# A recurrence, two mixture stages and a greedy routing on one core: the first two turns laid out anew, and the row numbers of an expert found a step sooner

## The reference, cut to what matters

```
for t in range(768):                       # 4 batches x 8 heads, head size 48
    y[t]  = r[t] . (state + u*k[t] (x) v[t])
    state = w[t]*state + k[t] (x) v[t]
x  = y as 3072 tokens x 384
h  = x @ w_in                              # 384 -> 2048
g  = h * tanh(softplus(h))
x2 = g @ w_out                             # 2048 -> 384
logits = x2 @ w_gate                       # 8 experts
# greedy routing: (token, expert) pairs by falling logit; a token keeps its
# first expert, an expert takes 384 tokens at most
out[tokens of e] = relu(x2[tokens of e] @ w1[e]) @ w2[e]
```

## Time and profile before

| | us |
|---|---|
| median of 3 runs (798.05 to 803.17) | 799.06 |
| the profiled execution | 798.34 |
| its span, first to last instruction | 796.6 |
| PE busy | 769.7 (97%) |
| DVE busy | 628.6 (79%) |
| ACT, POOL busy | 425.1, 292.7 |

### The profile page before, as it was taken

One profiled execution on the slowest core, in us unless ns is written; L12 is line 12 of the kernel. 1 busy time (PEld: TensorE's weight loads), 2 busy tenths in 40 slices (PEclk: granted clock), 3 DMA queues, 4 the chain that ended last, 5 costly groups with the idle time before them and its releaser, 6 DMA issues.

```text
span 796.6 us, 17145 instructions
## 1 busy us (share of the span) xinstructions
PE 769.7 (97%) x6810; PEld 577.1 (72%) x6810; DVE 628.6 (79%) x1081; ACT 425.1 (53%) x703; POOL 292.7 (37%) x244
## 2 busy tenths in 40 slices
PE   8899999999999999999999999987999999999994
PEld 8888878787878787878787877655565665666662
DVE  8969999999998999998999985877776767766220
ACT  2478759595968595868686779410121221222221
POOL 4424482627272727272726350011221231222311
PEclk9999999999999999999999999995999999999998
DMA  9962266464656464655464347114423415415500
GB/s 306 377 210 64 78 201 245 144 237 142 233 187 213 151 230 159 212 210 196 170 208 174 117 154 248 61 53 157 172 90 148 188 61 189 187 44 207 218 31 30
DMA packets 47791, 133.49 MB, mean 168 GB/s; under 512 B 5344, under 2 KB 19808, under 8 KB 45664
## 3 DMA queue, kind: packets, MB, share of 16 engines
q1 hardware_dynamic: 38880, 93.07, 33.7%
q0 software_dynamic: 5376, 34.61, 11.8%
q10 hardware_dynamic: 3456, 4.72, 1.7%
HBM read 97.78 MB, written 34.60 MB: 166 GB/s over the span
## 4 chain that ended last, share of the span: by engine, by line
PE 83%; DVE 10%; issue 2%; DMA 2%; ACT 2%; POOL 0%; SPq 0%; DVEq 0%
PE bank L425 80%; DVE cmp L1316 2%; DMA stage<-in_moe_w_out 1%; DVE g_lo L1416 1%; ACT t_sb L807 1%; PE bank L730 1%; PE bank L450 1%; PE bank L511 1%; DVE inv L1008 1%; DMA k_tok<-in_k 1%; DVE t_sb L1395 1%; DVE rdec L1023 0%; DVE t_sb L1388 0%; DVE t_sb L1391 0%; DVE thr L1333 0%
## 5 line engine op out<-in xcount | busy, mean ns | idle before, releaser
L425 PE MATMUL bank<-x_hi,win_hi 128*128 128x256 f16 (+1 forms) x588 | 158.8, 272 | 1.6 <-DVE h_sb L1080 0.9
L425 PE MATMUL bank<-x_lo,win_hi 128*128 128x256 f16 (+1 forms) x588 | 158.7, 272 | 0.0
L425 PE MATMUL bank<-x_hi,win_lo 128*128 128x256 f16 (+1 forms) x588 | 158.7, 272 | 0.0
L1547 POOL TENSOR_TENSOR g_lo<-t_sb,g_hi 128x512 f16<-128x512 f32 x88 | 122.3, 1420 | 47.0 <-ACT g_hi L807 47.0
L425 PE MATMUL bank<-wout_hi,g_hi 128*128 128x392 f16 (+1 forms) x416 | 129.0, 317 | 0.0
L425 PE MATMUL bank<-wout_lo,g_hi 128*128 128x392 f16 (+1 forms) x416 | 128.8, 316 | 0.0
L425 PE MATMUL bank<-wout_hi,g_lo 128*128 128x392 f16 (+1 forms) x416 | 128.7, 316 | 0.0
L807 ACT ACTIVATE g_lo<-bank 128x384 f16<-128x384 f32 x64 | 31.4, 490 | 144.1 <-PE bank L425 124.7
L1530 POOL TENSOR_TENSOR dv<-v_tok,dot 128x384 f32<-128x384 f32 x24 | 29.8, 1240 | 186.7 <-DVE dot L1038 186.7
L807 ACT ACTIVATE g_hi<-t_sb 128x512 f16<-128x512 f32 x96 | 56.5, 624 | 54.6 <-PE bank L425 54.4
L1087 DVE TENSOR_TENSOR t_sb<-t_sb,h_sb 128x512 f32<-128x512 f32 x96 | 83.0, 913 | 2.0 <-ACT t_sb L807 1.4
(11 more groups left out here) (184 smaller groups left out, 1593.7 us busy)
## 6 DMA issues: line engine op xcount, KB each, us to landing
stage<-in_moe_w SPq DMA_DIRECT2D x22, 768.0 KB, 6.5
w_split<-stage SPq DMA_DIRECT2D x22, 768.0 KB, 4.5
fold_w<-in_moe_w SPq DMA_DIRECT2D x10, 768.0 KB, 8.9
w_split<-fold_w SPq DMA_DIRECT2D x10, 768.0 KB, 7.6
wt<-in_w_turned SPq DMA_DIRECT2D x24, 258.0 KB, 2.8
kt<-in_k_turned SPq DMA_DIRECT2D x24, 256.0 KB, 2.6
rt<-in_r_turned SPq DMA_DIRECT2D x24, 256.0 KB, 2.8
r_tok<-in_r SPq DMA_DIRECT2D x24, 192.0 KB, 6.0
```

What stands on the lines that cost most here:

```text
L425: return nc.tensor.matmul(*a, **k)
L1547: G.tensor_tensor(g_lo[:, j * GW:(j + 1) * GW], t_sb[:, j * GW:(j + 1) * GW], g_hi[:, j * GW:(j + 1) * GW], ALU.subtract).then_inc(s["glo" ...
```

## The change

- **PE, turns 0 and 1.** The blocks of folded products go: `fold_one` puts single ones between the matmuls of tiles (0,4), (0,5), (0,7), (1,3), (1,4) and of three half tiles, 42 in all, and 6 stand at the end of turn 0. `values(2)` goes between the matmuls of tile (0,6). The first halves of turn 1's tiles 0, 1 and 2 are made at the end of turn 0, as they need only chunk 2's x; `values(3)` goes between the matmuls of two of them. `scores(2)` moves behind tile (0,4). In turn 1 chunk 5's steps come two slots later.
- **DVE, turns 0 and 1.** A new list. `gated(0, 1)` to `gated(0, 7)` move from the end of turn 0 into slots 0 to 5 of turn 1, `split_piece(2)` moves ahead of `inverse(2, 0)`, `split_piece(4)` and `(5)` into turn 0. `copied` of turn 1 waits also for the product of the same part of h.
- **ACT, turns 0 and 1.** `rounded(0, ...)` moves into turn 1's slots 0 to 6, ahead of the copies; in turn 0 the pieces 4 and 5 come two slots later, and chunk 3's keys and x among the sines. POOL's `remainder(0, ...)` follow, and its piece 3 waits for one more DVE piece.
- **Second stage.** `PLACES`, DVE's loop and the idle products:

```diff
-        PLACES = {("A", 0): ["Y1"], ("B", 0): ["H4"], ("A", 1): ["I", "Y2"], ("B", 1): ["J", "H5"],
-                  ("A", 2): ["Y3"], ("B", 2): ["H6"], ("A", 3): ["Y4"], ("B", 3): ["H7"],
-                  ("A", 4): ["Y5"], ("B", 4): ["X", "Y6"], ("A", 5): ["Y7"],
-                  ("B", 5): ["H0", "H1"], ("C", 0): ["H2", "Y0", "H3"]}
+        PLACES = {("A", 0): ["Y4"], ("B", 0): ["H7", "Y5"], ("A", 1): ["Y6"], ("B", 1): ["Y7"],
+                  ("A", 2): [], ("B", 2): ["X"], ("A", 3): [], ("B", 3): ["H0", "H1"],
+                  ("A", 4): ["Y0"], ("B", 4): ["H2"], ("A", 5): ["Y1"], ("B", 5): ["H3"],
+                  ("C", 0): ["H4", "Y2", "I", "H5", "J", "Y3", "H6"]}
+        OLDER = ("Y4", "H7", "Y5", "Y6", "Y7")
...
-                p = r - 1 if u in YOUNG + ("I", "J") else r - 2
+                p = r - 2 if u in OLDER else r if u in ("I", "J") else r - 1
...
-                if r == 1:
-                    idle_products(16)
...
-                    if r == 1 and t < 4:
+                    if r == 1 and t < 2:
                         idle_products(6)
...
                 ranks(r)
-                units(r, ("C", 0), unit)
+                if r == 0:
+                    idle_products(8)
+                    unit(0, "I", 0)
+                    idle_products(8)
+                    unit(0, "J", 0)
+                    idle_products(12)
+                else:
+                    units(r, ("C", 0), unit)
...
+            def steps_of(r):
+                filled(r, 0)
+                next_step(r, 0)
+                low_h(r - 2, 7)
+                filled(r, 1)
+                next_step(r, 1)
+                filled(r, 2)
+                next_step(r, 2)
+                low_xg(r - 1)
+                filled(r, 3)
+                next_step(r, 3)
+                low_h(r - 1, 0)
+                filled(r, 4)
+                low_h(r - 1, 1)
+                next_step(r, 4)
+                filled(r, 5)
+                low_h(r - 1, 2)
+                choose(r)
...
             for r in range(E - 1):
+                steps_of(r)
+                low_h(r - 1, 3)
+                take_slots(r)
+                row_numbers()
+                low_h(r - 1, 4)
+                id_blocks(r)
+                pick_expert(slice(0, NT))
...
+                token_ids(r)
                 leave()
                 if r < E - 2:
                     start_search()
+                low_h(r - 1, 5)
+                low_h(r - 1, 6)
```

More of the change, by code:

```diff
@@ L513, in turn_x, with fold_one @@
                 last.then_inc(s["xT"], 1)
+            FOLDS = {(0, 4): 4, (0, 5): 7, (0, 7): 7, (1, 0, 0): 6, (1, 1, 1): 4, (1, 2, 1): 2, (1, 3): 6, (1, 4): 6}
+            to_fold = [(t, k3) for t in range(FT) for k3 in range(KT)]
+            def fold_one():
+                if len(to_fold) == FT * KT:
+                    pe.wait_ge(s["gload"], 16)
+                    pe.wait_ge(s["wotload"], 64)
+                t, k3 = to_fold.pop(0)
+                q, f = t // (FT // 4), t % (FT // 4)
+                last = mm(ab[0][:, t * E:(t + 1) * E], wot[q][:, k3, f * P:(f + 1) * P], w_gate[:, k3, :],
+                          start=k3 == 0, stop=k3 == KT - 1)
+                if f == FT // 4 - 1 and k3 == KT - 1:
+                    last.then_inc(s["fold"], 1)
             def tile(i, j, values_of=None, begin=0, end_at=0):
@@ L589, in finish, with half_tile @@
                 pass
[L591 to L605, removed]
+            def half_tile(i, j, c, values_of=None, begin=0, end_at=0):
+                if c == 0:
+                    if i == 0:
                         pe.wait_ge(s["whi"], 1)
@@ L622, in turn @@
                 n0, n1 = CH * (i + 1), CH * (i + 1) + 1
[L623 to L626, removed]
+                late = 2 if i == 1 else 0
+                between = {6: (n0, 0, 12), 7: (n0, 12, 16), 10 + late: (n1, 0, 12), 11 + late: (n1, 12, 16)}
+                if i == 0:
+                    between = {6: (n0, 0, 16)}
+                here = between.get(slot, ()) if i < NI - 1 else ()
+                if (i, slot) in ((0, 0), (0, 1), (1, 0), (1, 1), (1, 2)):
+                    half_tile(i, slot, 1)
                 elif slot < NJ:
@@ L636, in turn @@
                         keys(2)
[L637 removed]
                     elif slot == 6:
                         turn_x(2)
+                    elif slot == 7:
                         scores(3)
[L641 removed]
+                        half_tile(1, 0, 0)
                         keys(3)
[L643 removed]
+                        half_tile(1, 1, 0, 3, 0, 12)
+                        half_tile(1, 2, 0, 3, 12, 16)
                         turn_x(3)
[L645 to L646 removed]
+                        for _ in range(6):
+                            fold_one()
                     return
[L648 to L649 removed]
+                if i == NI - 1:
+                    return
                 if slot == 3:
@@ L1477, in _ @@
                     start_search()
-                    digits()
-                    numbered()
-                    low_h(new, 2)
+                low_h(r - 1, 5)
+                low_h(r - 1, 6)
             did(V.memset(mem[:, NT:2 * NT], 0.0))
@@ L1483, in _ @@
             prefixes()
-            low_h(E - 3, 2)
-            digits()
-            numbered()
-            low_h(E - 3, 3)
-            one_hot_low()
-            low_h(E - 3, 4)
-            id_blocks(E - 2)
-            token_ids(E - 2)
-            low_h(E - 3, 5)
             take_slots(E - 1)
-            digits()
-            numbered()
-            low_h(E - 3, 6)
-            one_hot_low()
             low_h(E - 3, 7)
+            row_numbers()
             low_xg(E - 2)
-            for f in range(6):
+            for f in range(5):
                 low_h(E - 2, f)
-                if f == 4:
-                    id_blocks(E - 1)
-                    token_ids(E - 1)
+            id_blocks(E - 1)
+            low_h(E - 2, 5)
+            token_ids(E - 1)
             low_h(E - 2, 6)
@@ L1560, in turn @@
                         own(n1)
+                elif i == 0:
+                    if slot == 8:
+                        diagonal(4)
+                        remainder(0, 0)
+                elif i == 1 and slot < 12:
+                    if slot == 5:
+                        own(4)
+                    elif slot == 8:
+                        diagonal(5)
+                    if 1 <= slot < NJ:
+                        remainder(0, slot)
+                    elif slot > NJ:
+                        remainder(1, slot - NJ - 1)
+                elif i == 1:
+                    if slot == 12:
+                        own(5)
+                    remainder(1, slot - NJ - 1)
+                    if slot == SLOTS - 1:
+                        remainder(1, NJ - 1)
                 elif slot == 0 and with_att:
```

218 lines of the change are left out of this document (138 added, 80 removed).

## The result

The changed kernel takes 834.99 us (median of 4 runs, 830.77 to 835.98) against 799.28 before: ratio 1.0427, interval 1.0396 to 1.0458. It is slower, as forecast, but by 36 us and not by 13. The profiled execution took 835.3 us (span 833.6).

The account below looks back on a forecast made before the run. PE, 97% busy, was taken as the bound, with DVE at 79%. Turns −6.5, step 1 −1.4, steps 2 to 6 +16.5 and tail +4.8 gave +13.4 on the profiled 798.34: 811.7 us (812 against the median), range 797 to 821.

Parts of the forecast that it names:

- Turns 0 and 1: First-stage turns: cheaper products, fewer waits and a fuller clock, less new waits, save 6.5 us.
- DVE's new list: Turn 1, chunk 3's low x to the folded product's low part: 21 us, from 61.4 to 82.5, or 84.9 beside POOL.
- the half-way form: Rival: holes cost 1.5 us a step and the turns give 9.2, so 799 us; chance 0.2.
- Step 1: Second stage's first search: units start 4.6 us earlier, less 1.6 for counts and 1.6 for new waits: 1.4 us gain.
- Steps 2 to 6: Second stage: waits in emptied places and at C add 3.3 us a step, 31.20 to 34.5; five steps +16.5.
- a rival with 0.15: Rival, steps 2 to 6: holes also lower the clock on H0 and H1, up to +1.7 a step, 820 us; chance 0.15.
- The tail: After the last search: `ranks(7)` 2.0 us late, X to H0 waits 1.4 each for experts 6 and 7; +4.8 us.

Follow-up runs that it names:

- E1: Turns 0 and 1 of the change, with the old places, VectorE order and idle products behind them: 794.76 us, ratio 0.9949 to the kernel before (chip A).
- E5: The changed kernel again, on chip B: 833.38 us.
- E9: The changed kernel once more, on chip C: 835.08 us.
- E10: E3 repeated on chip C: 824.49 us, ratio 1.0309 to the kernel before.
- E12: E1 with more idle products through step 1's search, on chip C: 794.97 us, ratio 0.9942 to the kernel before.
- E14: E3 again, on chip A: 818.80 us, ratio 1.0249 to the kernel before.
- E3: The changed kernel with useless products in the holes of rounds 2 and 3, steps 2 to 6: 820.43 us, ratio 1.0284 to the kernel before (chip A).
- E4: The changed kernel with units spread one place apart and low parts of X's copies moved: 812.2 us, ratio 1.0170 to the kernel before (chip A).
- E6: New turns, row numbers ahead of the pick, all units but I and J at their old places: 815.87 us, ratio 1.0225 to the kernel before (chip B).
- E2: Old turns 0 and 1 with the changed second stage: 835.36 us, ratio 1.0464 to the kernel before (chip A).
- E8: E1 with turn 1's folded remainder ahead of the split of piece 7, on chip B: 795.17 us, ratio 0.9947 to the kernel before.
- E11: E2 repeated on chip C: 835.68 us.

## Why the prediction was wrong

Right sign, wrong size: 811.7 against the profiled 835.3 is 23.6 us short, which the marks divide exactly.

- **Turns 0 and 1: 6.5 predicted, 3.0 in the profile, 4 in E1's medians.** The first sums began at 86.95 us, where I had 84.9. The term that was mis-sized is DVE's new list, from 61.4 to 82.5, or 84.9 beside POOL: it began at 62.6, as chunk 3's low x came later, and ended at 86.6. I had given the shared rate to `gated` alone (three took 3.84 us). `key_side` and `query_side` of chunk 4 took 1.19 and 1.64 us beside GpSimd (0.69 each without it) and a scan 2.19 (1.22 without it), while reciprocals and copies from PSUM kept their 1.75 and 0.68. The folded remainder stood behind a 1.75-us split. The sums lost 1.0 more (20.42 for 19.45) and the turns behind them 0.5. The clock fell in neither turn here, as predicted; but five of the eleven other profiles with the new turns (E5, E9, E10, E12, E14) have a low stretch of 3.4 us in the first sums. (Two sums were off by a little: seven `gated` beside POOL, at my own 0.65 each, leave 4.6 and not 3 to 4; the half-way form is 800 and not 799.)
- **Step 1: −1.4 predicted, +1.5 measured.** X, H0 and the rounds came in my order; PE's wait for the first `full` was 2.6 us, where I had 0.35, by the late release. H0 began at 549.99, where I had 544: 3.5 of it from the turns, 2.3 from that wait.
- **Steps 2 to 6: +16.5 predicted, +28.6 measured.** The list of waits was right: E3, with full clock and prompt releases, has 34.53 us a step against my 34.5 (my terms add up to 3.2, not 3.3). The step that failed is that the sum took these holes for waits only and gave the lower clock nothing; it stood in the forecast as a rival with 0.15, and there at up to 8 us. Five steps of E10 take 176.3 us and those of the changed kernel 186.6; 10.3 us is the low clock (with two extra late releases in round 3 in it). The late releases, which I did not have, add 3.6. The five clean steps, 172.7, are 1.9 us under my 174.6, because step 2 of before was itself 2.1 us longer than the others.
- **Why I gave the clock 0.15.** I took X's transposes for work that keeps it up, and judged from one stretch in turn 1. The rule that I cited, the Trainium skill's "TensorE: Matmul & The Clock Gate", section "HAM oscillation", is the one the trace bears out: 0.50 in each step, on H0 and H1, directly behind the holes. It has the clock fall in every pass, which one step of E5 does not show. The rival with it, 820, was itself too low: it added to my sum one stretch of 3.4 us a step, where one of five is 6.8 here, two in E5 and four in E9, and none in the tail.
- **The tail: +4.8 predicted, +9.9 measured.** `ranks(7)` waited 1.56 where I had 2.0, but the 1.1 of `ranks(6)` and its I were not in my tail. From X to the unit behind it passed 3.46 us, 0.98 before: 2.5 each for my 1.4, twice: I had ACT free for X's copies, and Y7, directly ahead of X, gives it three copies of y first (1.25 us). E4, with X ahead of Y7, has no such wait. One low stretch cost 1.7 more. Together these are 9.3 of the 9.9.
- **What the change was bought with.** The row numbers ahead of the pick cost 2.9 us a step when nothing else changes (E6), and E4, the same order with the units evenly laid, 2.5. Five units earlier are worth nothing in themselves, since every unit runs once either way; they could pay only by filling idle time in step 1, and there VectorE's chain had grown by 3.4 us.

## What to carry to other kernels

Price a hole in TensorE's list twice: by the wait, and by the products behind it at half clock; here the holes of a step, 3.3 us of waits, brought 1.6 to 2.5 us of lower clock on top. Where a serial engine closes a loop, work put ahead of the value that the loop needs is paid in every turn of it, whatever it makes ready sooner. And for each copy on the path look at what its own engine was given just before, and for each VectorE operation at whether GpSimd is running: here products of two SBUF tiles and scans took longer beside it, reciprocals and copies from PSUM did not.

## What the runs showed that was not expected

- **A release that depends on the chip.** While GpSimd issues indirect transfers, VectorE's `full` can start up to 2.4 us after the last count, with VectorE idle, and usually just after the last transfer is issued. What holds it up is not shown, only where it stands in time. It is so in both profiles of the first chip, in all four of chip B and all four of chip C, and in none of six on chip A, where two of the same programs (E2, E3) ran with the same transfers at the same places. It moves with the gathers: round 3 before the change and in E8 and E12, round 0 after it and in E6. Before the change units hid it; uncovered it cost 0.73 us a step.
- **The same step with and without the low clock.** In E5 one step of five kept the clock of 1.00 with the same holes as its neighbours, and in E11 another (35.18 us). The changed kernel's four runs on chip C lie 10.8 us apart, and with the holes filled 1.2. But on chip B they lie only 1.1 apart, and on chip A with the holes filled 5.0, so that holes make the time scatter is not shown.
